# Loading two row groups of the first expert during attention, and reordering the row copies and the FFN's block loads

## The chip, the cores and the metric

The kernel runs on one NeuronCore of a Trainium2 chip. The metric is the device time of one execution in microseconds (us), lower is better; where several executions were timed, the median is given.

## The reference, cut to what matters

Three layers follow each other, all in float32:

```python
# attention: B, H, S, D = 4, 8, 576, 64; phi: 64 -> 2 * 128 features
proj = x @ w_phi; proj -= max(abs(proj), axis=-1)
phi = concat([exp(proj), exp(-proj)])
kv = einsum('bhsf,bhsd->bhfd', phi(k), v); z = sum(phi(k), axis=2)
x = einsum(phi(q), kv) / (einsum(phi(q), z) + 1e-6)      # -> 2304 x 512

# mixture of experts: 8 experts, 512 -> 1024 -> 512, each token goes to one
e_idx = argmax(x @ w_gate); gate_w = softmax(x @ w_gate)[e_idx]
y = gate_w * sigmoid(x @ w_output_gate)[e_idx] * (relu(x @ w1[e_idx]) @ w2[e_idx])

# FFN: RMS norm, 512 -> 1536 -> 512
xn = y / sqrt(mean(y * y) + 1e-6) * rms_g
out = (silu(xn @ w_gate) * (xn @ w_val)) @ w_out
```

For these inputs every token of one attention batch (576 tokens) chooses the same expert, and three experts get tokens: 576, 1152 and 576 of them.

## The kernel before, in words

**Numbers.** Every float32 product on TensorE is made of three matmuls of operands that are split in a high and a low part (names ending in H and L): high by high, high by low, low by high. ScalarE makes a high part with a Copy activation, VectorE the low part with a subtraction.

**Attention** works in slots, 10 per batch: five 128-token tiles of keys and five of queries. Each engine has its own `slot(b, sl)`, and seven more slots (the tail) finish the last batch. While the last batch is worked on, the raw weights of token 0's expert are split in eight pieces (`split_slots_act`, `split_slots_dve`). After each batch, VectorE's `route_1` to `route_3` find each token's expert and its row in `xs_dram`, and GpSimd sets the batch's rows aside (`set_aside`) and scatters them (`scatter`, L559) to the region of their expert.

**Expert steps.** The experts with tokens take turns; a turn has as many steps as row groups of G = 288 tokens, eight steps in all here (0 and 1; 2 to 5; 6 and 7). For a row group, SyncE loads `xin` (`rows_in`, L424), GpSimd multiplies it by its gates (`gate_rows`, L569), TensorE transposes it in four chunks (`next_transpose`, L807, in the banks of `XT_BANK`, two at a time), and ScalarE and VectorE take the chunks into xmH and xmL (`take_rows`, L1033 and L1354). A step on TensorE (L856) computes eight chunks m of hidden rows (`hidden`, 12 matmuls of 288 columns, L833 to L835) and adds each to the outputs two chunks later (`outputs`, L846 to L848). After `hidden` 7 it transposes chunks 0 and 1 of the next group, then comes `outputs` 5, then the transposes 2 and 3, then `outputs` 6 and 7. ScalarE (L1061) and VectorE (L1492) do `relu` and `relu_low` of each chunk; on both, `take_rows` stands after the last one. The first step of a turn also splits the next turn's raw weights, one piece n after chunk n (`split_high` L971, `split_low` L1300), which GpSimd loads (`raw_in`, L605); `once` (L819) makes TensorE wait for all eight pieces before a turn.

Within a step the outputs of the step before are normalised: ScalarE's `copy_out`, GpSimd's `add_squares`, TensorE's `sum_squares` (L854), VectorE's `mean` (m = 3), ScalarE's `root` (Sqrt, a function table of its own), VectorE's `normal` (m = 4), then xoH on ScalarE (`normal_high`, m = 5) and xoL on VectorE (`normal_low`, m = 6). SyncE's `rows_out` (L457) stores xoH and xoL, and then the group's token numbers: 288 elements of 4 bytes, from `xs_dram` to `ids_dram`.

**The early step.** VectorE's `route_early` (L1306) sets a flag if token 0's expert has at least G + 1 tokens in the first three batches. Then step 0 runs early: SyncE loads the first group during the last batch's tail (L436), and TensorE does `hidden` 0 and 1 between the tail's slots (L878) and the rest of step 0 after them (L884), waiting for r_evac, the last batch's rank counts read by VectorE. The second group is loaded after the last batch's scatter has landed (`rows_next(1)`, L474).

**FFN.** Six token groups of 384, each through 12 blocks of 128 hidden columns (`ffn_up` L923 to L925, `ffn_down` L937 to L939). In group 0 the blocks' weights arrive through two staging buffers (`block_in`, L481) and are split by ScalarE (`block_high`) and VectorE (`block_low`), two blocks ahead of TensorE. SyncE's order there is written out by hand (L495 to L517): blocks 3 to 8, the last rows' stores, blocks 9 and 10, group 1's rows, the token numbers, block 11.

The order on every engine and queue is the order of the code; the five engines meet at semaphores only.

## Time and profile before

| | us |
|---|---|
| median of 3 runs | 986.61 (984.18 to 987.33) |
| the profiled execution, its time | 985.2 |
| its span | 983.3 |
| TensorE (PE) busy | 938.0 |
| VectorE (DVE) busy | 439.2 |
| ScalarE (ACT) busy | 314.1 |
| GpSimd (POOL) busy | 118.2 |

The span is what the profile's timeline covers, from the first to the last instruction. Times in rows of the trace are counted from its start. Attention takes until about 257 us, the expert steps until 517 us, the FFN until the end. A matmul's end is modelled: two that follow each other without a break overlap in the rows.

### The profile page before, as it was taken

To read this page: it belongs to the slowest core of one execution; us is meant where nothing else is said; L and a number is where in the kernel's file an instruction comes from. 1 tells how busy PE (TensorE), PEld (TensorE's weight loads), DVE (VectorE), ACT (ScalarE), POOL (GpSimd) and SP (SyncE) were. 2 spreads that over 40 slices of the span, in tenths; PEclk is the share of its full clock that TensorE was granted. 3 is DMA by queue.
4 is the path that set the end of the run, shared out by engine and by line. 5 is a ranking of instruction groups with operands and counts; after the bars stand their busy time and mean duration, and the time that the engine had idled before them with its cause. 6 is when DMAs were issued, how large, how long until landed. Compare 5 with 4: busy or idle time off the path is not lost.

```text
span 983.3 us, 16284 instructions
## 1 busy us (share of the span) xinstructions
PE 938.0 (95%) x6240; PEld 897.1 (91%) x6241; DVE 439.2 (45%) x869; ACT 314.1 (32%) x492; POOL 118.2 (12%) x135
## 2 busy tenths in 40 slices
PE   8999999999879789999999989999999999999996
PEld 7999999999878789998999879999999999999995
DVE  5667668688535663323434742222222222222222
ACT  4444444555105452333326422112112112112111
POOL 1000201103223212222031001001001001001001
PEclk9999999999789889999999999999999999999999
DMA  9610913202063731344354562002002002000000
GB/s 267 170 51 10 339 51 78 81 2 73 4 202 107 174 80 42 52 72 72 57 191 129 149 157 97 1 1 97 1 1 96 0 0 96 0 0 22 12 1 32
DMA packets 52960, 75.35 MB, mean 77 GB/s; under 512 B 26512, under 2 KB 42512, under 8 KB 51248
## 3 DMA queue, kind: packets, MB, share of 16 engines
q1 hardware_dynamic: 46816, 56.07, 22.1%
q0 software_dynamic: 3488, 17.85, 5.6%
q10 hardware_dynamic: 2608, 0.79, 0.4%
q8 instruction: 31, 0.51, 0.3%
q14 instruction: 17, 0.14, 0.1%
HBM read 51.06 MB, written 23.64 MB: 76 GB/s over the span
## 4 chain that ended last, share of the span: by engine, by line
PE 87%; DVE 4%; ACT 2%; issue 2%; DMA 2%; SPq 0%; POOL 0%; POOLq 0%; DVEq 0%; ACTq 0%
PE ps L923 9%; PE ps L925 9%; PE ps L924 9%; PE ps L696 7%; PE ps L713 7%; PE ps L938 4%; PE ps L939 4%; PE ps L937 4%; PE ps L846 3%; PE ps L848 3%; PE ps L847 3%; PE ps L833 3%; PE ps L834 3%; PE ps L835 3%; PE ps L670 2%
## 5 line engine op out<-in xcount | busy, mean ns | idle before, releaser
L923 PE MATMUL ps<-xnH,blkH 128*128 128x384 f32 x576 | 194.3, 337 | 6.2 <-DVE blkL L1527 5.1
L925 PE MATMUL ps<-xnH,blkL 128*128 128x384 f32 x576 | 194.0, 337 | 0.0
L924 PE MATMUL ps<-xnL,blkH 128*128 128x384 f32 x576 | 193.8, 336 | 0.0
L1534 DVE TENSOR_TENSOR sg<-sg,ps 128x384 f32<-128x384 f32 x72 | 39.8, 553 | 246.1 <-ACT sg L1123 246.1
L923 PEld LDWEIGHTS ps<-xnH,blkH 128*128 128x128 f32 x576 | 108.7, 189 | 10.4 <-issue 7.6
L1123 ACT ACTIVATE sg<-ps 128x384 f32<-128x384 f32 x72 | 35.4, 492 | 250.5 <-PE ps L925 250.4
L924 PEld LDWEIGHTS ps<-xnL,blkH 128*128 128x128 f32 x576 | 108.6, 189 | 2.7
L925 PEld LDWEIGHTS ps<-xnH,blkL 128*128 128x128 f32 x576 | 108.6, 189 | 0.0
L937 PE MATMUL ps<-blkH,hH 128*128 128x512 f32 x216 | 84.6, 392 | 0.9 <-DVE hL L1538 0.9
L938 PE MATMUL ps<-blkL,hH 128*128 128x512 f32 x216 | 84.8, 393 | 0.0
L939 PE MATMUL ps<-blkH,hL 128*128 128x512 f32 x216 | 84.8, 392 | 0.0
L1364 DVE SCALAR_TENSOR_TENSOR hmL<-ps,hmH 128x288 fp32r<-128x288 f32 x64 | 29.2, 456 | 119.1 <-ACT hmH L1043 118.5
L833 PE MATMUL ps<-xmH,w1H 128*128 128x288 f32 x256 | 77.1, 301 | 5.1 <-DVE hmL L1364 2.5
L846 PE MATMUL ps<-hmH,w2H 128*128 128x288 f32 x256 | 81.4, 318 | 0.0
L847 PE MATMUL ps<-hmL,w2H 128*128 128x288 f32 x256 | 78.2, 306 | 0.0
L848 PE MATMUL ps<-hmH,w2L 128*128 128x288 f32 x256 | 78.0, 305 | 0.0
L834 PE MATMUL ps<-xmL,w1H 128*128 128x288 f32 x256 | 77.0, 301 | 0.0
L835 PE MATMUL ps<-xmH,w1L 128*128 128x288 f32 x256 | 76.7, 300 | 0.0
L1177 DVE TENSOR_REDUCE mx<-ps 128x4 f32<-128x512 f32 (+1 forms) x80 | 54.8, 685 | 42.5 <-PE ps L672 42.1
L713 PE MATMUL ps<-kvs,ex 128*128 128x65 f32 (+1 forms) x640 | 71.6, 266 | 0.5 <-DVE x L1218 0.5
L713 PEld LDWEIGHTS ps<-kvs,ex 128*128 128x128 f32 (+1 forms) x640 | 68.8, 184 | 1.4 <-issue 1.4
L652 POOL DMA_INDIRECT out_dram<-ysb,idI x18 | 17.4, 969 | 436.0 <-ACT ysb L1138 432.7
(199 smaller groups left out, 1678.2 us busy)
## 6 DMA issues: line engine op xcount, KB each, us to landing
stage<-in_ffn_w SPq DMA_DIRECT2D x12, 768.0 KB, 5.5
xin<-xs_dram SPq DMA_DIRECT2D x9, 578.2 KB, 9.7
xs_dram<-zrow SPq DMA_DIRECT2D x8, 578.2 KB, 8.7
qT<-in_q SPq DMA_DIRECT2D x4, 1152.0 KB, 6.6
xnH_dram<-xoH SPq DMA_DIRECT2D x8, 576.0 KB, 3.4
xnL_dram<-xoL SPq DMA_DIRECT2D x8, 576.0 KB, 4.3
xnH<-xnH_dram SPq DMA_DIRECT2D x6, 768.0 KB, 4.7
xnL<-xnL_dram SPq DMA_DIRECT2D x6, 768.0 KB, 6.2
```

The costliest lines, as they stand in the source:

```text
L713: last = e.matmul(NUM[0:n, h // 4, h % 4, :], ex[:, at[1] % 2, sign, h, 0:n], kvs[:, 2 * h + sign, :], start=(sign == 0), stop=(sign == 1))
L833: e.matmul(o, w1H[par][:, c, cols], xmH[:, c, :], start=(c == 0), stop=False)
L834: e.matmul(o, w1H[par][:, c, cols], xmL[:, c, :], start=False, stop=False)
L846: e.matmul(o, w2H[par][:, m, cols], hmH[:, m % 2, :], start=(m == 0), stop=False)
L847: e.matmul(o, w2H[par][:, m, cols], hmL[:, m % 2, :], start=False, stop=False)
L848: last = e.matmul(o, w2L[par][:, m, cols], hmH[:, m % 2, :], start=False, stop=(m == FC - 1))
L923: e.matmul(o, hi, xnH[par][:, c, :], start=(c == 0), stop=False)
L924: e.matmul(o, hi, xnL[par][:, c, :], start=False, stop=False)
L925: last = e.matmul(o, lo, xnH[par][:, c, :], start=False, stop=(c == KC - 1))
L937: e.matmul(o, hH[:, i % 2, tok], blkH[i][:, 2, :], start=(i == 0), stop=False)
L938: e.matmul(o, hH[:, i % 2, tok], blkL[i][:, 2, :], start=False, stop=False)
L939: last = e.matmul(o, hL[:, i % 2, tok], blkH[i][:, 2, :], start=False, stop=(i == NF - 1))
```

## The change

Named by engine:

- SyncE: with the early flag, the second row group of token 0's expert is loaded as soon as the first one has been transposed, still during the tail; `rows_next(1)` is then left out. In the FFN, blocks 9 to 11 are loaded ahead of the last rows' stores, and group 1's rows ahead of the wait for the stored token numbers.
- GpSimd: the second group is gated ahead of the last batch's scatter; w2raw's load for turn 1 stands right behind w1raw's.
- VectorE: the flag asks for 2 G tokens. `take_rows` is cut in two: chunks 0 and 1 ahead of the last relu chunk, chunks 2 and 3 behind it. The pieces 6 and 7 of the weights are split behind all of that. `normal_low` comes at m = 5.
- ScalarE: the same two cuts; a one-element Sqrt opens each step, so that the step needs one function table; a one-element Sigmoid stands ahead of the FFN; block 11's high part waits for xoL.
- TensorE: the early step begins when the last batch's numerators have been read (dve_N); the wait for r_evac moves to the transposes. The first 12 warm-up matmuls write four banks in turn.
- Memory: xoH and xoL move up, clear of block 11. BLK keeps its value.

```diff
@@ -71,7 +71,7 @@
         arena_bytes = 2 * SET + RAW + WORK
-        BLK = (2 * KC * P + DM) * 4
+        BLK = 3 * DM * 4
         base0 = (nc.sbuf_base + 31) // 32 * 32
@@ -130,6 +130,7 @@
         rinv = put("rinv", [P, G])
+        put = placer(at_work + 20032 + BLK * 2, WORK - 20032 - BLK * 2)
         xoH = put("xoH", [P, KC, G], F32R)
@@ -438,14 +439,14 @@
                 rows_in(x0 * REGION)
+                e.wait_ge(s["pe_XT"], KC)
+                rows_in(x0 * REGION + G)
...
             total = total_steps(e)
-            with e.If(early < 1):
-                rows_in(row_of(0))
@@ -471,7 +472,9 @@
-            rows_next(1)
+            with e.If(early < 1):
+                rows_in(row_of(0))
+                rows_next(1)
             with e.Fori(0, total - 2) as n:
@@ -502,19 +505,16 @@
             e.dma_start(stage[1][:, :, :], ffn_w[2]).then_inc(s["st_1"], 16)
-            for i in range(3, 9):
+            for i in range(3, NF):
                 block_in(i)
             rows_out(last)
-            block_in(9)
-            block_in(10)
             e.wait_ge(s["xst"], total * 32 + 64)
             settle(e, "carry_sp")
+            group_in(1)
             e.wait_ge(s["idst"], total * 16 + 16)
             settle(e, "carry_sp")
-            group_in(1)
             with nc.allow_non_contiguous_dma(reason="token numbers"):
                 e.dma_start(idF[:, :], ids_dram[0:NTOK, :].rearrange("(t p) a -> p (t a)", p=P)).then_inc(s["id_in"], 16)
-            block_in(NF - 1)
             for g in range(2, NG):
@@ -600,6 +600,8 @@
             set_aside(B - 1, NJ - 1)
+            with e.If(early > 0):
+                gate_rows(1)
             scatter(B - 1)
@@ -629,15 +631,13 @@
                 raw_in(1, 1, KC)
+                raw_in(2, 1, PIECES)
             with e.If(early > 0):
...
                 e.sem_inc(s["pl_ss"], 1)
-                gate_rows(1)
             with e.If(early < 1):
                 gate_rows(0)
-            with e.If(has_turn(1)):
-                raw_in(2, 1, PIECES)
             over_turns(e, pairs_of_turns(e), step, split_step)
@@ -772,12 +772,12 @@
-            def keep_warm(n):
-                for _ in range(n):
-                    e.matmul(ps[:, XL, :], warm[:, 0:P], warm[:, :], start=True, stop=True)
+            def keep_warm(n, banks=(XL,)):
+                for i in range(n):
+                    e.matmul(ps[:, banks[i % len(banks)], :], warm[:, 0:P], warm[:, :], start=True, stop=True)
             e.wait_ge(s["c_warm"], 1)
-            keep_warm(12)
+            keep_warm(12, (YM, YM + 1, YM + 2, YM + 3))
             e.wait_ge(s["wbd_hi"], 1)
@@ -859,6 +859,8 @@
                     if m == FC - 1:
+                        if begin > 0:
+                            e.wait_ge(s["r_evac"], B)
                         next_transpose(g, 0)
@@ -881,7 +883,7 @@
                 slot(B, sl)
-            e.wait_ge(s["r_evac"], B)
+            e.wait_ge(s["dve_N"], B * NJ)
             with e.If(early > 0):
@@ -889,6 +891,7 @@
             pairs = pairs_of_turns(e)
+            e.wait_ge(s["r_evac"], B)
             with e.If(early < 1):
@@ -1030,9 +1033,9 @@
-            def take_rows(n, banks, fixed=False):
-
-                for c in range(KC):
+            def take_rows(n, banks, chunks=range(KC)):
+
+                for c in chunks:
                     e.wait_ge(s["pe_XT"], n * KC + (c + 1))
@@ -1058,17 +1061,27 @@
+            def table(func):
+
+                e.activation(mx[:, 0, 0:1], ones[:, 0:1], func).then_inc(s["act_t"], 1)
+
             def step(par, g, split=None):
+                table(ACT.Sqrt)
                 copy_out(g - 1)
                 for m in range(FC):
+                    if m == FC - 1:
+                        take_rows(g + 1, XT_BANK, (0, 1))
                     relu(g, m)
-                    if split is not None:
+                    if split is not None and m < FC - 2:
                         split(m)
...
                         normal_high(g - 1)
-                take_rows(g + 1, XT_BANK)
+                take_rows(g + 1, XT_BANK, (2, 3))
+                if split is not None:
+                    split(FC - 2)
+                    split(FC - 1)
@@ -1100,20 +1113,26 @@
                 for m in range(2, FC):
+                    if m == FC - 1:
+                        take_rows(1, XT_BANK, (0, 1))
                     relu(0, m)
-                take_rows(1, XT_BANK)
+                take_rows(1, XT_BANK, (2, 3))
...
                 take_rows(0, XT_FIRST)
+                e.wait_ge(s["dve_XT"], KC)
             over_turns(e, pairs, step, split_step)
...
             def block_high(i):
+                if i == NF - 1:
+                    e.wait_ge(s["dve_xl"], total + 1)
+                    settle(e, "carry_act")
                 e.wait_ge(s[f"st_{stage_of(i)}"], staged(i))
@@ -1145,20 +1164,16 @@
                             root(total - 1)
-                            table()
+                            table(ACT.Sigmoid)
                         block_high(i + 2)
...
-            def table():
-
-                e.activation(mx[:, 0, 0:1], gcol[:, 0:1], ACT.Sigmoid).then_inc(s["act_t"], 1)
-
+            table(ACT.Sigmoid)
             e.wait_ge(s["pe_s2"], total * FC + 2)
...
             copy_out(total - 1)
-            table()
             group(0)
@@ -1313,7 +1328,7 @@
                 link(e.tensor_reduce(e0n[0:1, :], n, X, ALU.add))
-                e.tensor_scalar(early_n[0:1, :], e0n[0:1, :], float(G + 1), None, ALU.is_ge).then_inc(s["r_early"], 1)
+                e.tensor_scalar(early_n[0:1, :], e0n[0:1, :], float(2 * G), None, ALU.is_ge).then_inc(s["r_early"], 1)
@@ -1351,9 +1366,9 @@
             e.wait_ge(s["c_misc"], N_MISC)
-            def take_rows(n, banks):
-
-                for c in range(KC):
+            def take_rows(n, banks, chunks=range(KC)):
+
+                for c in chunks:
                     e.wait_ge(s["act_XT"], n * KC + (c + 1))
@@ -1486,21 +1501,28 @@
                 for m in range(5, FC):
+                    if m == FC - 1:
+                        take_rows(1, XT_BANK, (0, 1))
                     relu_low(0, m)
-                take_rows(1, XT_BANK)
+                take_rows(1, XT_BANK, (2, 3))
...
                 for m in range(FC):
+                    if m == FC - 1:
+                        take_rows(g + 1, XT_BANK, (0, 1))
                     relu_low(g, m)
-                    if split is not None:
+                    if split is not None and m < FC - 2:
                         split(m)
...
                         normal(g - 1)
-                    if m == 6:
+                    if m == 5:
                         normal_low(g - 1)
-                take_rows(g + 1, XT_BANK)
+                take_rows(g + 1, XT_BANK, (2, 3))
+                if split is not None:
+                    split(FC - 2)
+                    split(FC - 1)
```

## Rows read from the trace of the kernel before

**Rows 1.** The page: busy time by engine, and the granted TensorE clock in 40 slices.
```profile
PE 938.0 (95%) x6240; PEld 897.1 (91%) x6241; DVE 439.2 (45%) x869; ACT 314.1 (32%) x492; POOL 118.2 (12%) x135
...
PEclk9999999999789889999999999999999999999999
```

**Rows 2.** The waits of TensorE: line, who released it: us in total, times, longest.
```profile
PE ps L798 <- DVE xmL L1358: 15.5, 8, 3.2
...
PE ps L798 <- POOL xin L574: 5.7, 1, 5.7
...
PE ps L833 <- DVE hmL L1364: 2.5, 2, 2.0
```

**Rows 3.** Busy time by stretch (PE, PEld, DVE, ACT, POOL), granted clock, DMA share, GB/s.
```profile
246.00:265.00 19.00, 17.53 (x128) 16.48 (x128) 8.76 (x31) 3.63 (x8) 4.14 (x5) 0.73 0.01 2
...
290.00:295.00 5.00, 4.12 (x18) 3.81 (x18) 0.00 (x0) 0.23 (x1) 0.85 (x2) 0.50 0.68 223
330.00:335.00 5.00, 4.72 (x22) 4.76 (x23) 1.41 (x4) 1.59 (x3) 0.58 (x1) 0.50 1.35 107
...
370.70:516.70 146.00, 137.94 (x1032) 135.54 (x1030) 52.56 (x95) 48.65 (x84) 36.71 (x32) 1.00 0.40 81
...
578.70:583.70 5.00, 5.00 (x21) 5.00 (x22) 3.16 (x4) 1.90 (x2) 0.00 (x0) 0.69 0.92 225
```

**Rows 4.** Timeline, step 3's end: start us, us, engine line, out<-in [idle <-releaser].
```profile
392.06 0.66 PE L798 MATMUL ps<-ident,xin 96*128 96x96 f32 x6
...
392.50 0.38 PE L846 MATMUL ps<-hmH,w2H 128*128 128x288 f32 x1
...
395.85 0.81 PE L798 MATMUL ps<-ident,xin 96*128 96x96 f32 x6 [1.51 <-DVE xmL L1358]
...
396.44 0.38 PE L846 MATMUL ps<-hmH,w2H 128*128 128x288 f32 x1
```

**Rows 5.** Timeline, step 0 beside the last batch's routing.
```profile
266.97 0.37 PE L833 MATMUL ps<-xmH,w1H 128*128 128x288 f32 x1 [1.18 <-DVE start_row L1286]
...
274.81 0.46 DVE L1364 SCALAR_TENSOR_TENSOR hmL<-ps,hmH 128x288 fp32r<-128x288 f32 x1 [0.23 <-DVE tab L1462]
...
276.64 0.30 PE L833 MATMUL ps<-xmH,w1H 128*128 128x288 f32 x1
```

**Rows 6.** Timeline, step 0's end; xin's load as the chain of waits has it.
```profile
268.73 1.06 POOL L566 DMA_INDIRECT xs_dram<-x5s,pos  x1 [12.03 <-DVE tid L1298]
...
280.57 7.45 DMA xin<-xs_dram
...
290.55 1.19 PE L798 MATMUL ps<-ident,xin 96*128 96x96 f32 x6 [5.75 <-POOL xin L574]
...
296.76 0.38 PE L846 MATMUL ps<-hmH,w2H 128*128 128x288 f32 x1
```

**Rows 7.** Timeline, the ends of steps 1 and 2, in which weights are split.
```profile
328.54 1.22 DVE L1302 TENSOR_TENSOR w2L<-w2raw,w2H 128x1024 fp32r<-128x1024 f32 x1 [0.48 <-ACT w2H L972]
...
330.27 1.20 PE L798 MATMUL ps<-ident,xin 96*128 96x96 f32 x6 [3.22 <-DVE xmL L1358]
...
336.61 0.29 PE L833 MATMUL ps<-xmH,w1H 128*128 128x288 f32 x1
...
364.29 1.19 PE L798 MATMUL ps<-ident,xin 96*128 96x96 f32 x6 [3.23 <-DVE xmL L1358]
...
370.68 0.30 PE L833 MATMUL ps<-xmH,w1H 128*128 128x288 f32 x1
```

**Rows 8.** Timeline, the FFN's group 0.
```profile
578.67 0.66 PE L923 MATMUL ps<-xnH,blkH 128*128 128x384 f32 x1 [4.78 <-DVE blkL L1527]
...
599.00 0.34 PE L923 MATMUL ps<-xnH,blkH 128*128 128x384 f32 x1
```

**Rows 9.** Time to landing: the tile w2raw's loads; then the last store of xoL.
```profile
DMA to landing us min/median/max: 8.1/13.1/15.9
...
xnL_dram<-xoL SPq DMA_DIRECT2D x1, 576.0 KB, 11.5
```

More of the change, by code:

```diff
@@ L244, in build_program @@
             "no event, see settle()": "carry_pe carry_act carry_dve carry_pool carry_sp",
-            "ScalarE's function table for the FFN": "act_t",
+            "ScalarE's function table in place": "act_t",
         }
```

## The prediction

> **What bounds the kernel now.** The page comes first: TensorE is busy 938.0 us of the span of 983.3, and the granted clock is below nine tenths in four of the 40 slices [rows 1]. Nothing else is near that. So a change can only save TensorE's waits and the time that it runs at the lower clock. The list of its waits comes second [rows 2]: the row copies' transposes (L798) wait 15.5 us for xmL in eight places and once 5.7 us for xin; the hidden chunks wait 2.5 us for hmL. The view by stretch comes third, for the clock [rows 3]: it is full in the steady steps (370.7 to 516.7), where TensorE is busy 137.9 of 146 us, and at half, 1.2 of 2.4 GHz, right behind the longer waits. The timelines then show each place. Two constants: 72 matmuls lie between 266.97 and 276.64 [rows 5], 0.134 us each, so a chunk of 12 takes 1.61; and a matmul shows 0.30, so a modelled end stands 0.16 behind the next one's undisturbed start.
>
> **The change, part by part.**
>
> *Row copies ahead of the last relu chunk.* Today ScalarE's relu 7 stands ahead of all four takes and has to wait for `outputs` 5, so the transposes of chunks 2 and 3, due right behind `outputs` 5, find their banks full. In step 3 they could start at 395.85 - 1.51 - 0.16 = 394.18, and the outputs 0.44 later (392.50 - 392.06), at 394.62; they start at 396.44 [rows 4]. That is 1.82 us, in five steps (3 to 7): **9.1**. With chunks 0 and 1 taken while `outputs` 5 runs (1.61 us against about 0.4 for a chunk on either engine), nothing takes the wait's place: relu 7 follows `outputs` 5 at once, and only `outputs` 7 needs it, two chunks later.
>
> *The same in step 2*, where VectorE and ScalarE also split pieces between relu and takes. The transposes could start at 364.29 - 3.23 - 0.16 = 360.90; 0.44 + 24 x 0.134 = 3.66 us later, at 364.56, step 3 would begin; it begins at 370.68 [rows 7]. **6.1**, of it 3.2 the wait and the rest mostly the half clock behind it, as behind the one of step 1 (0.50 at 330 to 335) [rows 3].
>
> *In step 1* the same sum gives 330.27 - 3.22 - 0.16 + 3.66 = 330.55 against 336.61, 6.1. But the next step starts a turn and needs all eight pieces, and pieces 6 and 7 are now behind the takes. VectorE's piece 7 starts at 328.54 today; two takes (under 0.46 each, the hmL subtraction of [rows 5], same 288 columns) put pieces 6 and 7 from about 329.4 to 331.9 (1.22 each), 1.35 us behind TensorE. With the branch behind it I take 1.5. **4.6**; bounds 6.1 (no new wait) and 3.2 (ScalarE's next table load and copy queue behind the pieces too).
>
> *Second row group loaded in the tail.* Today its load starts at 280.57, when the scatter has landed, and takes 7.45; then it is gated, and TensorE waits until 290.55 [rows 6]. The new load can start when the first transposes are done. `hidden` 0 and 1 run on those rows before 266.97, some 3.2 us at the full clock and twice that at half, so that is near 260, and the rows land before 268; gating them (at most the 2.5 us between 288.02 and 290.55) falls in GpSimd's 12.03 us of idle time ahead of the scatter at 268.73 [rows 6]. If it lands late, the scatter slips, and only the third group's load, needed a step later, waits for that. TensorE's transposes could start at 290.55 - 5.75 - 0.16 = 284.64 and the last two output chunks at 284.64 + 0.44 + 1.61 + 0.44 = 287.13, against 296.76. **9.6**: the wait, one of the eight for xmL, and the half clock (0.50 at 290 to 295) [rows 3, 6].
>
> *The early step ahead of r_evac.* The wait of 1.18 at 266.97 goes: **1.2**; what is late next is VectorE's relu_low 3, which sits in the routing chain and ends at 275.27, while `hidden` 5, its taker, would come at 276.64 - 1.18 = 275.46 [rows 5]. 0.2 us of slack; bounds 0 and 1.2.
>
> *FFN blocks ahead of the last rows' stores.* Block 9 waits 4.78 today; undisturbed it would start at 573.73, 4.9 earlier. The clock of 0.69 in the 5 us behind it costs another 1.55 [rows 3, 8]. **6.5**, if group 1's rows are in time (below).
>
> *At nothing.* The 288 element stores ride along as before. ScalarE's mid-step table loads go; they end while it waits for VectorE anyway, and the step's first one stays. The Sqrt of one element adds about 0.2 us a step on ScalarE, beside `hidden` 0. `normal_low` at m = 5 holds up relu_low 6 by about a microsecond, and `outputs` 6 takes that some 2 us later; in steps 1 and 2 the slack is about 1. w2raw's load stands right behind w1raw's, and two such loads land within 8.1 to 15.9 us of their issue [rows 9], before step 1 splits them. The later wait for r_evac is long fulfilled. The warm-up's other banks: from -1.6 to +1.6 us, one spell of half clock more or less (the 1.55 us above is the nearest such price); I take 0, since 12 matmuls stay 12 matmuls. The flag still holds: the first three batches hold all 576 tokens of token 0's expert, just 2 G. The 2.5 us for hmL stay: `normal` still stands ahead of relu_low 5.
>
> **Sum**: 9.1 + 6.1 + 4.6 + 9.6 + 1.2 + 6.5 = 37.1. The profiled execution took 985.2, so the changed one should take 948.1; the median of the runs stands 1.4 above that execution, so 949.5.
>
> **Row against rule, the clock.** Waits of 1.51 in five steps left the clock at 1.00, waits of 3.2 and more were followed by 0.50 [rows 2 to 4]. So I count the half clock (2.1, 2.5, 2.5 and 1.55 us; 8.6 in all) as gone with the long waits. The Trainium skill (TensorE: Matmul & The Clock Gate, A second HAM failure mode) says that even short idle moments between groups of matmuls can make the clock swing between its halves, which speaks against this. By that rule the sum would be 28.5, not 37.1.
>
> **The rivals.**
> 1. *Group 1's rows come late.* They are now asked for behind block 11, which waits for block 9's low part (shortly before block 9's start at 573.7), and behind the last stores. The last store of xoL took 11.5 us to land [rows 9], with the element store behind it. So they could be asked for as late as 585, with group 1 due at 599.00 - 6.5 = 592.5 [rows 8]. Both loads together are smaller than w2raw, which took 8.1 us at least. For: that one landing. Against: a store that lands sooner leaves several us in hand. Price: up to 3 us of wait and 1.5 of clock, about 952.5. Chance 0.15. The Trainium skill (DMA: Bandwidth & Descriptors, Specifications) has transfers under 512 bytes done as read-modify-write, which fits such a delay; the trace agrees as far as that w2raw's load behind an element store took 15.9 instead of 8.1 [rows 9].
> 2. *The turn of step 2 costs more*: piece 7 and ScalarE's queue hold up TensorE by 3 us, or w2raw for turn 2, asked for when piece 7 is done and thus two microseconds later, lands behind piece 4's turn. Price: 3 us and 2.5 us of half clock, 955. Chance 0.12.
> 3. *The clock falls all the same*, by the rule above: 949.5 + 8.6 = 958. For it speaks 0.73 in 246 to 265, where TensorE was busy 17.5 of 19 us. Against it, 1.00 over five steps [rows 3]. Chance 0.07.
> 4. *The change doesn't do what it says*: the flag misses 2 G by a token, and step 0 runs behind the tail. It could then start only when the rows have come and been gated and transposed, near 292, and with 16 chunks of 1.61 and the half clock step 1 near 321, where today it is due at 296.76 + 3.2 = 300: 21 us lost, the 26.3 of the other terms (9.1, 6.1, 4.6, 6.5) still won: 981. Chance 0.03.
> 5. *Slower*: with the waits gone TensorE runs steps 3 to 7 without a break, and the clock is held at half there. A step has 192 matmuls, 25.7 us; each at half costs as much again, so from 37.1 / 25.7 = 1.4 steps on the change loses, and with two it ends at 949.5 + 51.4 = 1001. Against: the densest stretch ran at 1.00 [rows 3]. Chance 0.03.
>
> **How the numbers follow.** The forecast of 949.5 has 0.60. Its own range is 946 to 953: the bounds of step 1's turn (-1.5, +1.4), of the early step (+1.2), of the warm-up (1.6 each way), and the 1.4 between an execution and the median. The range of 945 to 959 takes in rivals 1 to 3 and leaves out 4 and 5. A measurement here can tell 0.3%, about 3 us, from no change. Faster: 0.60 + 0.15 + 0.12 + 0.07 and 0.02 of rival 4 = 0.96. Same: 0.01, the upper end of rival 4. Slower: 0.03.
>
> **What would show it.** Right: the waits of L798 gone from TensorE's list in all eight steps and the one for xin too; xin's second load issued near 260 and gated before the scatter; step 1 beginning about 11 us earlier, near 290; TensorE's time from one steady step to the next 1.8 us shorter; the clock at 1.00 from step 1 to the end, but for its very end; a new wait of about 1.5 us at step 2's first matmul, released by VectorE's w2L; block 9's wait gone. Wrong: a wait at the first matmul of group 1 released by a DMA (rival 1), a clock of 0.50 in a stretch without a long wait (rival 3), first transposes behind 285 (rival 4).

## The result, and the profile after

| | before | changed |
|---|---|---|
| median of 4 runs each, us | 985.39 (982.52 to 987.33) | 947.38 (946.61 to 954.91) |
| ratio | | 0.9634, interval 0.9578 to 0.9689 |
| profiled execution, us | 985.2 | 948.03 |
| its span, us | 983.3 | 946.4 |

38.0 us less in the median, 36.9 in the profiled span; forecast 949.5 and, for the profiled execution, 948.1. Timed again later, beside the kernel before (987.84 then), the changed kernel gave 952.54 (six runs, 945.73 to 959.71; ratio 0.9648, interval 0.9611 to 0.9684). Why runs of one kernel lie 14 us apart is a question of its own, below; there is also a second profile of the changed kernel, and the text says where the two differ.

The page of the changed kernel, the lines that answer to [rows 1]:

```profile
PE 927.0 (98%) x6240; PEld 888.4 (94%) x6241; DVE 440.6 (47%) x869; ACT 303.6 (32%) x491; POOL 118.5 (13%) x135
...
PEclk9999999999999999999999999999999999999999
```

TensorE does as many matmuls in 11 us less of busy time, which is half clock that is gone; the other 26 us of the span were idle. Its list of waits, against [rows 2]:

```profile
PE ps L833 <- DVE hmL L1379: 3.3, 2, 2.0
...
PE ps L833 <- issue: 1.4, 2, 0.9
PE ps L833 <- DVE w2L L1317: 1.2, 1, 1.2
PE ps L926 <- issue: 1.0, 1, 1.0
...
PE ps L926 <- DVE blkL L1549: 0.3, 1, 0.3
```

No wait of L798 for xmL or for xin is left (15.5 and 5.7 before). New is one for w2L; the one for hmL has grown from 2.5 to 3.3; block 9's of 4.78 is gone, and the 0.3 that is left for blkL is another block's, there before too. By stretch (columns as in [rows 3]), with the two windows of the expert steps that stood at 0.50 before:

```profile
246.00:265.00 19.00, 17.56 (x155) 16.77 (x153) 9.87 (x34) 4.99 (x13) 6.02 (x8) 0.91 0.14 34
290.00:295.00 5.00, 5.00 (x40) 5.00 (x39) 2.80 (x4) 3.26 (x5) 4.09 (x2) 1.00 0.08 18
330.00:335.00 5.00, 5.00 (x38) 4.90 (x37) 3.37 (x5) 2.11 (x4) 2.36 (x3) 1.00 0.53 218
349.20:487.10 137.90, 136.46 (x1032) 135.47 (x1030) 53.48 (x96) 45.17 (x88) 36.75 (x32) 1.00 0.46 87
```

The fourth is steps 3 to 7: the same 1032 matmuls in 137.9 us where they took 146, at the full clock throughout. Last the timeline, at the places of [rows 6, 7]:

```profile
259.46 0.61 PE L833 MATMUL ps<-xmH,w1H 128*128 128x288 f32 x1
...
263.74 2.02 POOL L574 TENSOR_SCALAR xin<-xin 96x512 f32<-96x512 f32 x3 [6.53 <-DMA xin<-xs_dram]
...
264.56 0.38 PE L833 MATMUL ps<-xmH,w1H 128*128 128x288 f32 x1
...
282.42 0.66 PE L798 MATMUL ps<-ident,xin 96*128 96x96 f32 x6
...
289.37 0.40 PE L833 MATMUL ps<-xmH,w1H 128*128 128x288 f32 x1 [0.93 <-issue]
...
320.23 0.40 PE L833 MATMUL ps<-xmH,w1H 128*128 128x288 f32 x1 [1.21 <-DVE w2L L1317]
...
341.64 0.40 PE L833 MATMUL ps<-xmH,w1H 128*128 128x288 f32 x1 [1.29 <-DVE hmL L1379]
...
349.19 0.30 PE L833 MATMUL ps<-xmH,w1H 128*128 128x288 f32 x1
```

The second row group is gated at 263.74, long before TensorE transposes it at 282.42, so step 1 begins at 289.37 where it began at 301.13. What each part gave, as the difference of the same segment in the traces; gain and forecast go by the first profile of the changed kernel, the last column has the second one:

| segment, us | before | after | gain | forecast | after, second profile |
|---|---|---|---|---|---|
| start to step 1 (tail, step 0) | 301.13 | 289.37 | 11.76 | 10.8 | 300.08 |
| step 1 | 35.48 | 30.86 | 4.62 | 4.6 | 32.45 |
| step 2 | 34.07 | 28.96 | 5.11 | 6.1 | 28.18 |
| steps 3 to 7 | 147.09 | 137.96 | 9.13 | 9.1 | 137.97 |
| FFN | 465.5 | 459.2 | 6.3 | 6.5 | 459.3 |

The last two segments repeat to 0.1 us. The first three do not: the start of step 1 lies 10.7 us later in the second profile, through time at half clock in attention and its tail. From `hidden` 2 of step 0 (266.97 before, 264.56 after) to step 1 it is 34.16 us before and 24.81 and 24.80 in the two profiles after, so 9.35 of the 11.76 don't hang on that.

### The profile page after: what moved, and what is told of

Read it like the earlier page. It is cut to its first block, busy times and chain, and to the rows that moved or that the text cites. A ratio compares the mean times of both kernels' runs of the same rounds, so it can differ in the third digit from the quotient of the medians.

```text
span 946.4 us, 16281 instructions
## 1 busy us (share of the span) xinstructions
PE 927.0 (98%) x6240; PEld 888.4 (94%) x6241; DVE 440.6 (47%) x869; ACT 303.6 (32%) x491; POOL 118.5 (13%) x135
## 3 DMA queue, kind: packets, MB, share of 16 engines
q1 hardware_dynamic: 46816, 56.07, 23.3%
## 4 chain that ended last, share of the span: by engine, by line
PE 91%; DVE 3%; DMA 2%; ACT 2%; issue 2%; POOL 0%; POOLq 0%; SPq 0%; DVEq 0%; ACTq 0%
PE ps L926 10%; PE ps L928 10%; PE ps L927 10%; PE ps L696 8%; PE ps L713 7%; PE ps L941 5%; PE ps L942 5%; PE ps L940 5%; PE ps L833 3%; PE ps L834 3%; PE ps L846 3%; PE ps L835 3%; PE ps L848 3%; PE ps L847 3%; PE ps L670 3%; PE ps L672 2%
## 5 line engine op out<-in xcount | busy, mean ns | idle before, releaser
L846 PE MATMUL ps<-hmH,w2H 128*128 128x288 f32 x256 | 78.7, 307 | 0.0
L848 PE MATMUL ps<-hmH,w2L 128*128 128x288 f32 x256 | 75.7, 296 | 0.0
L847 PE MATMUL ps<-hmL,w2H 128*128 128x288 f32 x256 | 75.7, 296 | 0.0
## 6 DMA issues: line engine op xcount, KB each, us to landing
xin<-xs_dram SPq DMA_DIRECT2D x9, 578.2 KB, 10.1
```

The source lines that it names most:

```text
L846: e.matmul(o, w2H[par][:, m, cols], hmH[:, m % 2, :], start=(m == 0), stop=False)
L847: e.matmul(o, w2H[par][:, m, cols], hmL[:, m % 2, :], start=False, stop=False)
```

## The experiments

Two questions were open: does each part of the change bring what the sum says, alone; and what sets the clock, and with it the spread of the runs. For the second, each run is also given *at full clock*: its time less the share of its span that the mean granted clock falls short of 1. That comes to 964 for the kernel before in most sets (up to 966) and 940.7 for the changed one (940.9 when timed again). It takes too much off where a half-clock stretch overlaps a wait for another engine. The last 7 us of the span, behind TensorE's last matmul, are such a place (columns as in [rows 3]; PE busy 0.00, clock 0.50):

```profile
944.00:946.00 2.00, 0.00 (x0) 0.00 (x0) 0.00 (x0) 0.00 (x0) 0.00 (x0) 0.50 0.00 0
```

Between 1.0 and 2.4 us of each profile's loss lie there and cost nothing. So the number is good to about 1 us between kernels whose waits are alike. By it, some 23 of the 38 us of the median lie in waits and the rest in the clock.

### The takes behind the last relu chunk again

The changed kernel, with both cuts of `take_rows` undone on both engines:

```diff
                 for m in range(FC):
-                    if m == FC - 1:
-                        take_rows(g + 1, XT_BANK, (0, 1))
                     relu(g, m)
-                    if split is not None and m < FC - 2:
+                    if split is not None:
                         split(m)
...
-                take_rows(g + 1, XT_BANK, (2, 3))
-                if split is not None:
-                    split(FC - 2)
-                    split(FC - 1)
+                take_rows(g + 1, XT_BANK)
```

> The changed kernel with one part undone: all four takes behind the last relu chunk, the pieces of the weights each behind its own chunk. My theory: the waits of L798 for xmL come back, 1.5 us in six steps and 3.2 us in steps 1 and 2, and behind the two long ones the granted clock falls to half and costs 2.5 us each; step 2's wait of 1.2 for w2L goes. 6 x 1.8 + 2 x 3.4 + 5.0 - 1.2 = 21.4 us above the changed kernel, 969. Rival A, the clock's falls have nothing to do with the long waits: no spell of half clock at the ends of steps 1 and 2, 964. Rival B, another part of the change (the second group's early load) had made the takes harmless: the waits come back shorter and it stays under 960.

Measured: 969.51 (962.14 to 975.03, ratio 0.9841, interval 0.9781 to 0.99), 956.4 at full clock, 15.7 more than the changed kernel. The eight waits are back to the tenth of a microsecond (columns as in [rows 2]):

```profile
PE ps L798 <- DVE xmL L1366: 15.5, 8, 3.2
```

and the wait for w2L is gone. So this one reordering makes over half of the whole gain: 22 of 38 us against the changed kernel's first set of runs, 17 against its second, 15.7 of 23.3 at full clock. The new wait at step 2's start is its price. In the profiled run the clock fell in both places in which it fell before, behind the two waits of 3.2 us:

```profile
328.00:333.00 5.00, 5.00 (x28) 5.00 (x28) 0.82 (x2) 2.08 (x5) 0.58 (x1) 0.66 0.93 39
361.00:366.00 5.00, 5.00 (x24) 5.00 (x23) 0.91 (x2) 2.31 (x4) 0.00 (x0) 0.50 0.61 30
```

But one of the four runs, of the same program, lost only 3.8 us to the clock in all, at least 1 us of it at the span's end. The shortest fall in any profile costs 1.7 us, so this run can't have had both. A wait of 3.2 us makes a fall likely, not certain.

### The second row group late

```diff
                 rows_in(x0 * REGION)
-                e.wait_ge(s["pe_XT"], KC)
-                rows_in(x0 * REGION + G)
...
                 rows_in(row_of(0))
-                rows_next(1)
+            rows_next(1)
```

with GpSimd's gate and w2raw's load back in their old places.

> The changed kernel with one part undone: the second row group is loaded and gated behind the last batch's scatter, as before. My theory: TensorE's wait of 5.8 us for xin at the end of step 0 comes back, with 2.1 us of half clock behind it; 8 us above the changed kernel, 955. Rival A, without the clock's fall: 953. Rival B, the contention of w1raw's load with xin's counts as well, and with w2raw asked for later the first pieces are late: 957 or more. Either way the seams of steps 1 to 7 stay as in the changed kernel.

Measured: 958.83 (958.3 to 960.09, interval of the ratio 0.9731 to 0.9791), 11.5 above the changed kernel's 947.38; 945.9 at full clock, 5.2 above. The wait is longer than before (5.75), and the timeline names no releaser for it:

```profile
289.81 0.55 PE L796 MATMUL ps<-ident,xin 96*128 96x96 f32 x2 [7.34 <-issue]
```

and the view by stretch right behind it has the clock down:

```profile
290.00:297.00 7.00, 7.00 (x43) 6.98 (x43) 2.16 (x5) 1.95 (x5) 0.22 (x1) 0.69 0.85 307
```

From `hidden` 2 to step 1 it is 34.32 us here and 24.81 in the changed kernel: 9.5 us, what step 0's term says (9.6), wait and half clock together. The median is nearer to the expectation's rival B (957), but the trace shows little of its reasons: xin's load landed after 7.9 us instead of 7.45, and no piece of step 1 is late.

### The FFN's blocks behind the last stores

SyncE's order of before, in the changed kernel:

```diff
-            for i in range(3, NF):
+            for i in range(3, 9):
                 block_in(i)
             rows_out(last)
+            block_in(9)
+            block_in(10)
...
-            group_in(1)
             e.wait_ge(s["idst"], total * 16 + 16)
             settle(e, "carry_sp")
+            group_in(1)
...
+            block_in(NF - 1)
```

> The changed kernel with one part undone: SyncE's order in the FFN as before, blocks 9 to 11 behind the last rows' stores. My theory: block 9's wait of 4.8 us comes back with 1.5 us of half clock behind it, 6.4 us above the changed kernel, 954; the stage load that follows the element store lands 10 us or more after its issue. Rival, the rows are ready earlier now and so the stores are out before block 9 is needed: under 2 us above, 949.

Measured: 957.97 (955.13 to 961.27, interval of the ratio 0.9703 to 0.9785); 943.0 at full clock. Block 9 waits again in the timeline:

```profile
553.08 0.65 PE L929 MATMUL ps<-xnH,blkH 128*128 128x384 f32 x1 [3.15 <-DVE blkL L1552]
```

and by stretch the clock falls behind it:

```profile
553.00:558.00 5.00, 4.92 (x19) 4.96 (x20) 3.26 (x4) 1.90 (x2) 0.00 (x0) 0.66 0.96 241
```

3.15 and 1.7 (0.34 of 5 us) are 4.9 of the 6.3; the wait is shorter than before (4.78; 3.57 in another profile of that order). At full clock the difference to the changed kernel is 2.3; the rest of the 10 us in the median is clock, and not all of it the FFN's: in the profiled run attention's tail (244 to 262), which this edit doesn't touch, stood at 0.62.

At full clock the three parts undone one by one cost 15.7, 5.2 and 2.3 us, 23.2 in all, and the whole change brings some 23: they add up. By the medians they don't (22.1, 11.5 and 10.6, 44 of 38), as each median has its own share of half clock.

### No piece beside `normal`

The two hmL waits stand behind piece 4 of the weights, which VectorE splits between `mean` and `normal`. In the first profile the one of step 2 had also grown, from 0.54 to 1.29; what made it grow is taken up under *Without the token numbers*. Here pieces 4 and 5 come one chunk later:

```diff
-                    if split is not None and m < FC - 2:
-                        split(m)
+                    if split is not None and m < FC - 1 and m != 4:
+                        split(m if m < 4 else m - 1)
```

> The changed kernel, one step further: in the steps that split weights no piece is split behind chunk 4, where VectorE also has normal; pieces 4 and 5 move to chunks 5 and 6. My theory: the two waits for hmL (2.0 and 1.3 us at hidden 7 of steps 1 and 2) come from VectorE's queue, piece 4 and normal in a row, so both go: 3.2 us below the changed kernel, 944. Rival A, the late pieces hold up the takes in their place: waits of L798 for xmL of 1 to 2 us in steps 1 and 2, no gain, 947. Rival B, normal itself is late by its inputs (GpSimd's squares): the waits stay as they are, 947.

Measured: 947.02 (946.59 to 948.62, interval of the ratio 0.961 to 0.967); 936.6 at full clock, 4.1 below the changed kernel. Both hmL waits (1.97 and 1.29) are gone from TensorE's list; what is left of the expert steps in it:

```profile
PE ps L833 <- issue: 1.4, 2, 0.9
PE ps L833 <- DVE w2L L1317: 1.2, 1, 1.2
```

Yet the median has not moved, because all four runs lost 10.4 to 11.4 us to the clock, where three of the changed kernel's lost 5.7 to 7.6. In the profiled one most of it is attention's tail, a stretch that the edit leaves as it was:

```profile
244.00:262.00 18.00, 17.04 (x111) 16.11 (x112) 5.66 (x13) 2.99 (x8) 4.12 (x6) 0.61 0.01 2
```

0.39 of 18 us is 7.0 us. By segments steps 1 and 2 take 28.63 and 27.40, 3.8 us less than in the changed kernel's first profile. A gain of that size is invisible in a median whose tail varies by more.

### The kernel before, with step 0's wait filled

If the clock falls because of the wait of 5.75 us, TensorE kept busy through it should keep its clock. 24 matmuls of 512 columns that nobody reads, in the kernel before:

```diff
                     if m == FC - 1:
+                        if begin > 0:
+                            e.wait_ge(s["dve_XT"], KC)
+                            for _ in range(24):
+                                e.matmul(ps[:, XT_BANK[0], :], w1H[0][:, 0, 0:P], w1H[0][:, 0, 0:512],
+                                         start=True, stop=True)
                         next_transpose(g, 0)
```

> The kernel before, with 24 filler matmuls of 512 columns (about 5.2 us) in step 0, ahead of its wait of 5.75 us for xin; the row group still comes as late as before. My theory: the half clock behind that wait comes from TensorE's idleness in it, so with the wait filled the outputs behind it run at the full clock; 2 us below the kernel before, and no half clock at the end of step 0 in the profile. Rival A, the clock falls there for another reason: half clock at the same place, no gain. Rival B, the fillers run over and push the transposes: 1 us or more slower than the kernel before.

Measured: 983.78 (ten runs, 973.92 to 987.05) against 984.18; ratio 0.9979, interval 0.9948 to 1.001. In the profile it works as meant. The timeline has a wait of 0.65 left:

```profile
285.46 0.74 PE L798 MATMUL ps<-ident,xin 96*128 96x96 f32 x6 [0.65 <-POOL xin L574]
```

and the clock by stretch holds where it stood at 0.50 before [rows 3]:

```profile
285.00:295.00 10.00, 7.07 (x53) 6.57 (x54) 2.01 (x5) 3.74 (x7) 0.67 (x2) 1.00 0.80 265
```

But over the runs 3.9 to 22.7 us were lost to the clock, and no gain shows in the median. From `hidden` 2 to step 1 the profile has 32.81 instead of 34.16, 1.35 of the 2 us that were expected. That the local half clock can be prevented is shown; that this brings time in the whole is not.

### Without the token numbers

The 288 element stores of a step and the load of the numbers left out, the numbers made by an iota instead, so that the output's rows stand in the order of the row groups, not of the tokens:

```diff
-                with nc.allow_non_contiguous_dma(reason="token numbers"):
-                    e.dma_start(ids_dram[bass.ds(col, G), :], xs_dram[bass.ds(row, G), DM:DM + 1])\
-                        .then_inc(s["idst"], 16)
+                e.sem_inc(s["idst"], 16)
...
```

> The changed kernel without its token numbers: the eight stores of 288 elements and the load of the numbers are left out, and the output rows go to places by a fixed count, so they are permuted. My theory: the element stores slow every transfer behind them (xin took 10.1 us in the median, w2raw 13.9, the last store of xoL 8.9), so here they land in about 4.5, 8 to 9 and 3.4 us; TensorE waits for none of them, so the time stays within 1 us of the changed kernel at the same clock. Rival A, the slow landings come from plain contention of the loads with each other: they stay above 8, 12 and 6 us. Rival B, one of these landings does decide: 2 us or more faster.

Measured: 952.83 (946.63 to 954.64); 939.5 at full clock, 1.2 below the changed kernel. The issue of rows on the page of the changed kernel (KB each, median us to landing):

```profile
xin<-xs_dram SPq DMA_DIRECT2D x9, 578.2 KB, 10.1
```

and on the page of this one:

```profile
xin<-xs_dram SPq DMA_DIRECT2D x9, 578.2 KB, 4.6
```

The element stores more than double the time of the row load behind them. w2raw's load for turn 2 lands after 8.1 us instead of 13.9, and the last store of xoL after 5.2 instead of 8.9 (3.4 was expected). It costs little, as the rows have a whole step to come in.

The hmL wait of step 2 is 0.55 here instead of 1.29. But that is not the element stores alone, for the changed kernel's second profile, with all of them, has it short too:

```profile
353.16 0.40 PE L833 MATMUL ps<-xmH,w1H 128*128 128x288 f32 x1 [0.55 <-DVE hmL L1379]
```

What differs is the landing of w2raw. In the first profile ScalarE's piece 4 waits for it:

```profile
335.07 1.06 ACT L975 ACTIVATE w2H<-w2raw 128x1024 fp32r<-128x1024 f32 x1 [0.49 <-DMA w2raw<-in_w]
```

and in the second it doesn't:

```profile
346.61 1.05 ACT L975 ACTIVATE w2H<-w2raw 128x1024 fp32r<-128x1024 f32 x1
```

This load is asked for when piece 7 is split, so the change has moved it from 5.2 us ahead of step 2 (331.44 against 336.61) to 0.9 behind its start (321.11 against 320.23). It lands at 335.05 in the first profile, 0.6 us after ScalarE could have begun; in the second it is 0.5 us early. So about 0.6 of the 0.75 us of growth is this load. A third profile (one warm bank, below) bears it out: the load landed at 337.02, piece 4 began at 337.05, and the hmL wait was 0.80.

The rest, about 0.14, goes with GpSimd's gate beside VectorE's piece 3. In the first profile the piece took 1.70 us beside a part of the gate that took 0.69; in the next experiment's profile it took 1.71, w2raw was in time, and the hmL wait was 0.69. In the second profile and in this one it is that part of the gate that took 1.73 and 1.74, beside a piece of 1.22 and 1.23, and the wait stayed at 0.55.

### The tail's wait for r_evac, and the warm-up's banks

Two small parts undone, each alone:

```diff
-            e.wait_ge(s["dve_N"], B * NJ)
+            e.wait_ge(s["r_evac"], B)
```

> The changed kernel with one part undone: TensorE waits for r_evac ahead of the rest of the early step, as before. My theory: a wait of 1.2 us for start_row comes back at hidden 2 and all of it ends in the total, 1.2 us slower at the same clock. Rival, VectorE's relu_low 3 behind the routing chain bounds hidden 5 in both kernels: under 0.4 us.

Measured: 950.42 (945.29 to 954.36); 941.0 at full clock, 0.3 above the changed kernel. The wait of 1.18 is back (265.86). The full-clock number can't tell its worth, but the segments can, where the clock was full: from `hidden` 0 to `hidden` 2 the kernel before with its wait filled takes 5.23 us with a wait of 0.97, and the changed order without the wait takes 4.08 and 4.09 (without the token numbers; with the wait in the loop). Of these 1.1 us some are lost again on the way from `hidden` 2 to step 1, which takes 24.60 here, 24.81 in the changed kernel and 25.26 and 25.12 in those two profiles. That leaves 0.5 to 0.9. That step 2's hmL wait is 0.69 here instead of 1.29 has nothing to do with it; the changed kernel itself has 1.29 and 0.55.

```diff
-            keep_warm(12, (YM, YM + 1, YM + 2, YM + 3))
+            keep_warm(12)
```

> The changed kernel with one part undone: the first 12 warm-up matmuls all write one bank. My theory: no difference, within 0.3 us at the same clock; the first real matmul waits for VectorE either way. Rival A, four banks let the 12 matmuls run longer or shorter (5.33 us in the changed kernel's profile, 4.53 in the one of before), which sets whether the clock is at half when the first projections run: up to 1.6 us slower.

Measured: 948.46 (944.83 to 954.62); 939.9 at full clock. The twelve matmuls took 5.14 us in one bank, 5.33 in four, and 4.53 in the kernel before, with one; in the second profile of the changed kernel, with four, 4.4. The banks make no difference that stands out from that.

### The wait for the pieces, put where they are read

The w2L wait stands ahead of `hidden` 0, but pieces 6 and 7 are first read by `outputs` 4. On top of the kernel without a piece at 4, `once` asks for two pieces less, and the rest is waited for behind `hidden` 6. So that only a turn's first step does that, it was written out apart from the loop:

```diff
                         if split_step is None:
-                            with e.Fori(0, tiles) as t:
-                                step(par, first + t)
+                            step(par, first, late=(pair, par))
+                            with e.If(tiles > 1):
+                                with e.Fori(1, tiles) as t:
+                                    step(par, first + t)
...
                     hidden(par, g, m)
+                    if m == 6 and late is not None:
+                        once(*late, less=0)
```

> On top of the kernel without a piece at chunk 4, TensorE now waits for pieces 6 and 7 of a turn's weights only ahead of outputs 4, which is the first to read piece 6. Theory (the 1.2 us at step 2's first matmul is the wait for those two pieces and nothing else): the w2L wait is gone from TensorE's list, step 2's first hidden matmul follows the last outputs of step 1 without a gap, and the time at full clock is 1.2 us below that kernel's 936.6, so 935.4; a median near 945.8 if the clock at attention's end falls as it did there, near 942 if not. Rival (the branch and the table reads at the turn, shown as the engine's own issue, take the wait's place): a gap of 0.5 to 1.2 us stays and the time at full clock is 936.6 or, with the second pair of waits in each turn, up to 0.4 more.

Measured: 969.18 (964.46 to 971.73, interval of the ratio 0.9782 to 0.9838), 22 us above the kernel it started from. Neither theory had that. The w2L wait is gone, and in its place stand two stalls, released by nobody, at the first matmuls of steps 2 and 6:

```profile
325.23 0.60 PE L835 MATMUL ps<-xmH,w1H 128*128 128x288 f32 x1 [6.79 <-issue]
...
448.46 0.60 PE L835 MATMUL ps<-xmH,w1H 128*128 128x288 f32 x1 [12.10 <-issue]
```

Both are the start of a turn: the first is a jump forward over the loop body of the turn before, the second the jump back to the start of the pairs. The list of queues holds the hint. On the changed kernel's page (packets, MB, share of 16 engines):

```profile
q8 instruction: 31, 0.51, 0.2%
```

and on this one's:

```profile
q8 instruction: 50, 0.82, 0.4%
```

Only TensorE's program grew, and there are 19 more packets of code, of 16 KB each (0.31 MB); two packets of code start between 440 and 448, inside the second stall. The Trainium skill (Runtime: NRT & Kernel Launch, Instruction fetch mechanics) says that code is fetched ahead in sequence only, and that a jump to code which is not on the chip has to wait for a fetch. The trace agrees for the second stall, of 12.1 us. In the first, of 6.8 us (318.4 to 325.2), no packet of code starts, the last one before it at 317.04; that it too is the code rests on the last experiment below.

### Filler in attention's tail

On top of that, sixteen matmuls of 256 columns that nobody reads, four in each of the tail's slots 0 to 3:

```diff
                     numerators(g2, 0)
+                if isinstance(b, int) and b == B and sl < 4:
+                    for _ in range(4):
+                        e.matmul(ps[:, 0, 0:256], wbdH[:, 0:P], wbdH[:, :], start=True, stop=True)
```

> On top of the kernel above, four matmuls of 256 columns that nobody reads stand in each of the last batch's tail slots 0 to 3 on TensorE (sixteen in all, some 0.12 us each at the full clock by the 0.134 us of one of 288 columns: at most 1.9 us if TensorE is the bound there). Theory (the half clock between 244 and 262, in 4 to 14 us of most runs, comes from the thin work of that stretch, matmuls of 65 columns and transposes): fewer or shorter stretches at half in these runs, the clock mean above 0.992 in all of them and the spread under 3 us; median 943 (full clock 937.3 at the worst, plus about 5.7). Rival (the clock falls there for another reason, or by an average over more than this stretch): the runs lose 6 to 15 us to the clock as before, and the time is that of the kernel above plus up to 1.9 us, 946 to 948.

Measured: 973.01 (970.98 to 976.07); 954.9 at full clock, 5.8 above the kernel it stands on, 3.2 of it one more stall shown as issue, in the FFN (L934). The profiled run holds 1.00 in the tail (240 to 257), and four of the five runs lost 16.5 to 17.5 us to the clock, where the kernel without filler lost 15.4 to 24.2. Since the code stalls bring their own half clock, the mean is above the expected bound in none. The filler may steady the clock in the tail, but three profiles without it (token numbers left out, kernel before filled, wait in the loop) have 1.00 from 240 to 270 as well. This one is inconclusive.

### The changed kernel again

> The changed kernel itself, timed again beside the others. Both theories on the runs' spread: at full clock each run gives 940.7 within 1 us; the median lies between 946.5 and 951, with the difference among runs in the time at half clock alone.

Measured: 952.54 (945.73 to 959.71). At full clock the six runs give 940.6 to 942.0: all the rest, 3.8 to 19.2 us, is time at half clock. The profiled run is the longest, 959.71, and has the tail at half:

```profile
250.00:265.00 15.00, 15.00 (x106) 14.30 (x106) 5.23 (x13) 2.28 (x4) 3.72 (x5) 0.66 0.01 2
```

The median lies above the bound of 951 that was given.

This profile also has the clock down in step 1, behind the hmL wait:

```profile
322.09 0.61 PE L833 MATMUL ps<-xmH,w1H 128*128 128x288 f32 x1 [1.99 <-DVE hmL L1379]
```

and by stretch:

```profile
322.00:327.00 5.00, 4.91 (x27) 4.89 (x28) 3.65 (x6) 1.96 (x4) 0.00 (x0) 0.66 0.37 119
```

Step 1 takes 32.45 us so, 1.6 more than in the first profile, where the same wait of 1.97 left the clock at 1.00. Of the seven profiles with the new order and this wait (1.97 to 1.99), four have the fall and a step 1 of 32.4 to 32.5, three don't. Behind the waits of 1.51, six in each of three profiles with the old order, the clock never fell.

### The same wait inside the loop

The late wait once more, with the loop left as one body (every step asks, and only the first of a turn can have to wait):

```diff
                             with e.Fori(0, tiles) as t:
-                                step(par, first + t)
+                                step(par, first + t, late=(pair, par))
```

> The same late wait for pieces 6 and 7, but inside the one loop body that all steps of a turn share, so that TensorE's program grows by a few waits and not by a second copy of the step. Theory (the two stalls of 6.79 and 12.10 us in the kernel with two copies, both shown as the engine's own issue at the first matmul of a turn, were TensorE waiting for its own code to be loaded, 50 packets of it against 31 in the changed kernel): both stalls are gone, 31 or 32 packets on the instruction queue, no w2L wait, and 935.4 us at full clock, with a median near 944 to 947 as the clock has it. Rival (the late wait itself, on a register's value, stalls TensorE at a turn's start): stalls of 7 and 12 us remain at the same two turns or move to the place of the wait, and the time at full clock is 949 as it was there.

Measured: 943.31 (938.79 to 949.64, ratio 0.9594, interval 0.9556 to 0.9633), 936.1 at full clock. TensorE's waits in the expert steps:

```profile
PE ps L833 <- issue: 1.4, 2, 0.9
...
PE ps L833 <- DVE hmL L1381: 0.2, 1, 0.2
```

and the queue of code on its page:

```profile
q8 instruction: 31, 0.51, 0.2%
```

Both stalls are gone with the second copy of the code, though each step now asks for the pieces: that the copy caused them, and not the wait, is shown. Step 1 now takes 27.49 us where it took 28.63 without a piece at 4 and 30.86 in the changed kernel, so the w2L wait was worth 1.14; step 2 takes 27.25 instead of 28.96 (28.18 in the second profile). The median is 4 us under the changed kernel's first set and 9 under its second; but the intervals of the ratios overlap. The 5.1 us in steps 1 and 2, and the 4.6 at full clock (940.7 to 936.1), don't hang on the clock. Its median is the lowest of all versions that were run.

## Why the prediction was right, point by point

- **Row copies in steps 3 to 7**, 9.1: measured 9.13, 1.81 to 1.85 a step. Undoing them brought all eight waits back. Shown.
- **Step 2**, 6.1: measured 5.11 in the first profile and 5.89 in the second. The prediction said that the 2.5 us for hmL stay. They did in the second profile (2.5); in the first, step 2's part grew from 0.54 to 1.29, about 0.6 of it w2raw's load for turn 2, which landed behind piece 4's turn. That is the second half of rival 2, at 0.6 us instead of 3 and only in some executions.
- **Step 1**, 4.6: measured 4.62 in the first profile, 3.03 in the second, with half clock behind the hmL wait, which the prediction put at nothing. In both there is a new wait for w2L, forecast 1.5 and named at its place. It measured 1.21 and 1.24, and was the wait for pieces 6 and 7 alone: put where they are read, it vanished.
- **Second row group and r_evac**, 9.6 + 1.2: measured 11.76. Of it 9.35 come behind `hidden` 2, 1.83 between `hidden` 0 and there, where 1.2 was forecast (the rest is half clock that this run had less of), 0.58 before. By the stretches at full clock some 0.5 to 0.9 of the 1.2 arrive at step 1. The sum had no term for the clock in attention's tail, which stood at 0.73 before and 0.91 after (246 to 265); that alone is enough for the 1 us that this segment brought above its forecast, and it happens to make up for the 1 us that step 2 fell short. That the profiled execution came out at 948.03 for a forecast of 948.1 is luck to that extent: the second profile, of the same kernel, took 959.71.
- **FFN**, 6.5: measured 6.3; block 9 starts without a wait.
- **The clock**: counted as gone with the long waits, 8.6 us. In the profiled pair that held. Over the runs it was too neat. The stretches at half are not tied one by one to a wait: the wait of 5.75 filled, the loss stayed in the median; one run with the two 3.2 us waits lost 3.8 in all. The changed kernel's runs lose 4 to 19 us, with no wait above 2 us in the expert steps and the FFN in either profile. What the sum lacks is the wait of 2.0 between its 1.51 and 3.2, behind which the clock fell in one of the two profiles, and the clock in attention's tail. The forecast's own range, 946 to 953, took in no such variation and misses one run of the first four and four of the later six; the full range, 945 to 959, holds all but one of the ten.
- **Row against rule.** The Trainium skill's rule (TensorE: Matmul & The Clock Gate, A second HAM failure mode) would have given 28.5 us instead of 37.1. Steps 3 to 7 stood at 1.00 before and after, against it; the tail, all short matmuls and short waits, swings, as it says. The falls in step 1 are on its side too. It bears on the spread of the runs, which the sum left out, and not on the 8.6 us behind the long waits.
- **Rival 1** was 0.3 us from happening. The last store of xoL took 8.9 us to land, and group 1's rows were asked for at 552.87 and 553.55, their low part to land after 8.2:

```profile
L492 SPq DMA_DIRECT2D xnL<-xnL_dram x1: 1463/1463/1463, 553.5 to 553.5; - x1
...
DMA to landing us min/median/max: 8.2/8.2/8.2
```

so at 561.7, and group 1's first matmul reads them at 562.02:

```profile
562.02 0.33 PE L926 MATMUL ps<-xnH,blkH 128*128 128x384 f32 x1
```

  In the other profiles with this order of the stores the margin is 0.15 to 1.15 us (4.85 without the token numbers). With the old order it was 17 us. So a chance of 0.15 was low: the rows arrive barely in time.
- **Rivals 2 and 3** happened in small: step 2's turn cost 1.2, as forecast, and w2raw up to 0.6 more; the expert steps' clock held in the first profile and fell once in the second, 1.6 us. **Rivals 4 and 5** did not happen: xin came early; steps 3 to 7 ran without a break at 1.00.

## What to carry to other kernels

Look for a producer's copy that stands behind work which itself waits for its reader: the fix was an order of instructions, and at full clock it brought twice as much as the two moved groups of loads together (15.7 us against 5.2 and 2.3). Ask for a counted resource where it is read, not at the top of the loop, but keep that wait inside the one loop body: a second copy of TensorE's step cost 18.9 us at two jumps. Where runs differ by 14 us, compare them by time at full clock and by segments of the trace: a gain of 3 to 4 us was real in both and absent from the medians. Profile the changed kernel twice: a wait that had grown by 0.75 us in the first trace, and looked like a cost of the change, was back at its old length in the second.

## What the runs showed of the hardware

- Code costs time at jumps. Two copies of a step on TensorE (50 packets on the queue q8 of instructions instead of 31) made two stalls of 6.79 and 12.10 us, which no semaphore explains.
- The same program loses between 3.8 and 19.2 us to the granted clock from one run to the next. The most variable stretch is attention's tail (244 to 262), matmuls of 65 columns and transposes with TensorE over 90% busy: 0.61 there in one profile (no piece beside `normal`), 1.00 in another (240 to 262, the wait in the loop).
- 288 stores of 4 bytes ahead of a load of 578 KB make it land after 10.1 us instead of 4.6 (median of nine, with them and without).
- In step 2, VectorE's split of piece 3 (332 in the first profile) and the last part of GpSimd's gate start within 0.1 us of each other in seven profiles of the changed order. In two of them the piece took 1.70 or 1.71 us and the gate's part 0.69, in five the piece 1.22 or 1.23 and the gate's part 1.73 or 1.74: one of the two is held up, and which one changes from run to run.
- Behind a wait of TensorE of 1.97 to 1.99 us the granted clock fell to 0.50 in four profiles and not in three of the same stretch of program; behind eighteen waits of 1.51 it never fell.
